# Attention within a chunk of 128 tokens, made as two halves of 64, and y in eight tiles of the TensorE array

## What is computed

```python
# q, k, v, alpha: (batch 4, heads 8, tokens 768, 48)
for t in range(S):
    state = alpha[:, :, t, :, None] * state + einsum('bhd,bhde', k_t, v_t)
    y[:, :, t] = einsum('bhd,bhde->bhe', q[:, :, t], state)
x = y as 3072 tokens x 384
h = x @ w_in;   x = (h * tanh(softplus(h))) @ w_out     # moe, 384 -> 2048 -> 384
h = x @ w_in2;  out = (h * cos(h)) @ w_out2             # moe2, the same shapes
```

## Time and profile before

| | |
|---|---|
| Median of 3 runs | 895.30 us (895.29 to 895.43) |
| The profiled execution, its own time | 896.72 us |
| Its span, first to last instruction | 895.0 us |
| Mean granted TensorE clock | 0.999 of 2.4 GHz |
| PE busy | 882.7 us (99%), 5550 matmuls |
| DVE, ACT, POOL busy | 413.6, 408.7, 371.6 us (46, 46, 42%) |
| Instruction fetch | 0.72 MB in 44 transfers |

### The profile page before, as it was taken

The page is one execution under the profiler, slowest core; times in us unless marked ns, Lnnn a source line. Parts: engine busy times, 40 slices in busy tenths (PEclk is TensorE's granted clock), DMA queues, the critical chain, the costliest instruction groups (busy, mean ns, idle before and its releaser), DMA issues.

```text
span 895.0 us, 13987 instructions
## 1 busy us (share of the span) xinstructions
PE 882.7 (99%) x5550; PEld 729.4 (81%) x5550; DVE 413.6 (46%) x625; ACT 408.7 (46%) x702; POOL 371.6 (42%) x281
## 2 busy tenths in 40 slices
PE   8899999999999999999999999999999999999998
PEld 7688888888888888888878788888888888888886
DVE  8864422222233322221021666565666575666664
ACT  3534332223223222322345765565665565655554
POOL 3686454444444555442355423232323232323333
PEclk9999999999999999999999999999999999999999
DMA  9645221112122211210043200200200200100000
GB/s 212 179 146 146 67 74 40 39 39 75 39 52 59 81 39 40 74 30 1 36 129 101 89 1 0 71 1 1 70 1 1 72 1 0 71 1 1 35 1 36
DMA packets 17153, 48.13 MB, mean 54 GB/s; under 512 B 2752, under 2 KB 2752, under 8 KB 17088
## 3 DMA queue, kind: packets, MB, share of 16 engines
q1 hardware_dynamic: 17088, 47.23, 18.3%
HBM read 37.79 MB, written 9.44 MB: 53 GB/s over the span
## 4 chain that ended last, share of the span: by engine, by line
PE 94%; DVE 2%; DMA 1%; ACT 1%; issue 1%; POOL 0%; ACTq 0%; SPq 0%; DVEq 0%; POOLq 0%
PE bank L444 43%; PE bank L421 43%; PE bank L349 3%; PE bank L370 2%; PE bank L377 1%; PE bank L382 1%; PE bank L393 1%; PE bank L343 1%; DMA shared<-mid 1%; DVE growth L631 1%; DMA shared<-aqk_in 0%; DVE suffix L620 0%; ACT w_hi L486 0%; DVE w_lo L678 0%; ACT g L532 0%
## 5 line engine op out<-in xcount | busy, mean ns | idle before, releaser
L794 POOL TENSOR_TENSOR g_lo<-g,g_hi 128x512 fp32r<-128x512 f32 x192 | 258.3, 1346 | 471.4 <-ACT g_hi L525 471.4
L444 PE MATMUL bank<-g_hi,w_hi 128*128 128x512 f32 x576 | 226.9, 394 | 0.3 <-DVE x_out L694 0.3
L444 PE MATMUL bank<-g_hi,w_lo 128*128 128x512 f32 x576 | 224.3, 389 | 0.0
L525 ACT ACTIVATE g_hi<-g 128x512 fp32r<-128x512 f32 x192 | 120.7, 629 | 131.9 <-PE bank L444 131.2
L421 PE MATMUL bank<-x_hi,w_hi 128*128 128x512 f32 x576 | 162.5, 391 | 3.7 <-ACT g L532 2.2
L444 PE MATMUL bank<-g_lo,w_hi 128*128 128x512 f32 x576 | 166.0, 390 | 0.0
L421 PE MATMUL bank<-x_hi,w_lo 128*128 128x512 f32 x576 | 161.8, 389 | 0.0
L421 PE MATMUL bank<-x_lo,w_hi 128*128 128x512 f32 x576 | 161.8, 389 | 0.0
L421 PEld LDWEIGHTS bank<-x_hi,w_hi 128*128 128x128 f32 x576 | 107.7, 188 | 27.8 <-ACT g L532 3.4
L444 PEld LDWEIGHTS bank<-g_hi,w_hi 128*128 128x128 f32 x576 | 108.1, 188 | 24.8 <-issue 1.1
L539 ACT ACTIVATE shared<-bank 128x512 f32<-128x512 f32 x96 | 57.4, 598 | 154.1 <-PE bank L421 154.1
(11 more groups left out here) (79 smaller groups left out, 625.1 us busy)
## 6 DMA issues: line engine op xcount, KB each, us to landing
w_raw<-w_in SPq DMA_DIRECT2D x32, 384.0 KB, 3.3
shared<-aqk_in SPq DMA_DIRECT2D x44, 192.0 KB, 3.7
v_sb<-v_in SPq DMA_DIRECT2D x24, 256.0 KB, 4.2
shared<-aqk_in SPq DMA_DIRECT2D x48, 96.8 KB, 3.9
mid<-x_out SPq DMA_DIRECT2D x6, 768.0 KB, 5.5
shared<-mid SPq DMA_DIRECT2D x6, 768.0 KB, 6.0
out<-x_out SPq DMA_DIRECT2D x5, 768.0 KB, 4.0
out<-x_out SPq DMA_DIRECT2D x3, 256.0 KB, 2.4
```

What stands on the lines that cost most here:

```text
L444: mm = nc.tensor.matmul(acc[m][:, :], wp[:, f, DM + m * P:DM + (m + 1) * P], gp[:, tile % GB, :], start=(f == 0 and n == 0), stop=(f == FT ...
L525: nc.scalar.activation(g_hi[:, tile % GB, :], g[:, tile % GB, :], ACT.Copy).then_inc(ghi_ready, 1)
L794: nc.gpsimd.tensor_tensor(g_lo[:, tile % GB, :], g[:, tile % GB, :], g_hi[:, tile % GB, :].bitcast(F32), ALU.subtract).then_inc(glo_ready, 1)
```

## The change

A chunk is handled as two halves of 64 tokens. The scores are made within each half alone (64 x 64 instead of 128 x 128; half the masked product is not made any more). What the second half owes to the first comes through the state: `update(c)` now makes the sum of key·value for each half apart and stands ahead of `scores(c + 1)` and y; DVE adds the first half's sum to the state and has the state in the middle (`add_first`, `mid_state`), and later the second half's (`add_second`). y is made by `inner` (v·probs, 32 matmuls) and `outer` (state·q, 16 matmuls, twice), each on 64 rows and 32 columns of the array with 64 moving columns: eight tiles, two row halves by four column groups. The two row halves write different PSUM banks. In the second `outer` they change banks, so it waits for the first (`half_done`), and the transposes of the next chunk's keys (`turn`) stand between. An update is now made for the last four chunks too. The mask is one DVE instruction of the same 512 columns for a chunk, before two. PSUM is laid out anew: `first_product(1)` has a bank of its own, and after a chunk `first_product` waits for the copy of the turned keys instead of the state's addition. The first four chunks get four more ACT copies (`start_state`). `split_x2` comes two steps later, at steps 8, 10 and 12 of a block. Nothing is changed in the 3456 matmuls of the two feed-forward blocks. The diff, cut:

```diff
--- before.py
+++ after.py
...
+def next_scores_at(s):
     c = values_at(s)
     return c + 1 if c is not None and BATCH < c < CHUNKS - 1 else None
...
-    if BLOCKS <= j < 2 * BLOCKS and f in (6, 8, 10):
-        return j, (f - 6) // 2
+    if BLOCKS <= j < 2 * BLOCKS and f in (8, 10, 12):
+        return j, (f - 8) // 2
...
+        mid_state = sb("mid_state", [P, ST])
...
+        def h_of(tile):
+            if tile < TILES:
+                return sc[:, 0, :] if tile == 1 else h0[:, 0, :]
+            return (h0[:, 0, :], sc[:, 0, :], sc[:, 1, :], yu[:, 0, :])[tile % 4]
...
+        def y_of(c):
+            return acc3[:, 0:2, 0:DM // 2] if c in (1, 3) else yu[:, :, 0:DM // 2]
...
+        def update_of(c, half):
+            if half == 1 and c in (2, 3):
+                return acc3[:, 2, (c - 2) * PAIRS * D:(c - 1) * PAIRS * D]
+            return (acc3 if c in (1, 3) else yu)[:, half, DM // 2:DM // 2 + PAIRS * D]
...
+            def turn(c, s):
+                pe.wait_ge(kd_ready, c + 1)
+                if c > 0:
+                    pe.wait_ge(kdt_ready, c)
+                if c == BATCH:
+                    pe.wait_ge(xlo_ready, BATCH)
+                elif c > BATCH:
+                    pe.wait_ge(g_ready, s + 1)
+                for p in range(PAIRS):
+                    mm = nc.tensor.transpose(turn_of(c)[:, p * ROWS:(p + 1) * ROWS], k_of(c)[0:ROWS, p, :],
+                                             ident[0:ROWS, 0:ROWS])
+                mm.then_inc(keys_turned, 1)
...
                 for p in range(PAIRS):
-                    for i in range(2):
-                        rows = slice(64 * i, 64 * i + D)
-                        mm = nc.tensor.matmul((a, b)[i][:, p * P:(p + 1) * P], k_of(c)[rows, p, :],
-                                              q_of(c)[rows, p, :], start=True, stop=True)
-                        if p == PAIRS - 1:
-                            mm.then_inc(scores_done, 1)
...
+                    for half in range(2):
+                        t = slice(HALF * half, HALF * half + HALF)
+                        for i in range(2):
+                            rows = slice(64 * i, 64 * i + D)
+                            mm = nc.tensor.matmul(sc[t, i, p * HALF:(p + 1) * HALF], k_of(c)[rows, p, t],
+                                                  q_of(c)[rows, p, t], start=True, stop=True)
+                mm.then_inc(scores_done, 1)
+            def update(c):
...
+                pe.wait_ge(kdt_ready, c + 1)
...
+                    pe.wait_ge(sum_ready, min(c, UPDATES))
+                for p in range(PAIRS):
+                    for half in range(2):
+                        t = slice(HALF * half, HALF * half + HALF)
+                        for i in range(2):
+                            mm = nc.tensor.matmul(update_of(c, half)[64 * i:64 * i + D, p * D:(p + 1) * D],
+                                                  kd_t[t, c % 2, p, 64 * i:64 * i + D],
+                                                  v_sb[t, c % 3, 2 * p + i, 16 * i:16 * i + D], start=True, stop=True)
+                mm.then_inc(upd_done, 1)
...
+            def inner(c):
+                pe.wait_ge(probs_ready, c + 1)
+                if c >= BATCH:
+                    pe.wait_ge(mid_ready, c - BATCH + 1)
+                else:
+                    pe.wait_ge(first_state, c + 1)
+                for k in range(2):
+                    for half in range(2):
+                        t = slice(HALF * half, HALF * half + HALF)
+                        for n in range(4):
+                            nc.tensor.matmul(y_of(c)[32 * n:32 * n + 32, half, k * HALF:(k + 1) * HALF],
+                                             v_sb[t, c % 3, 2 * n + k, 32 * k:32 * k + 32], probs[t, c % 2, k, n, :],
+                                             start=(k == 0), stop=False, skip_group_check=True)
+                for i in range(2):
+                    for half in range(2):
+                        t = slice(HALF * half, HALF * half + HALF)
+                        for n in range(4):
+                            nc.tensor.matmul(y_of(c)[32 * n:32 * n + 32, half, 2 * HALF:3 * HALF],
+                                             v_sb[t, c % 3, 2 * n + i, 32 - 32 * i:64 - 32 * i], probs[t, c % 2, i, n, :],
+                                             start=False, stop=False, skip_group_check=True)
+            def outer(c, swapped):
+                if c >= BATCH:
...
+                for k in (None, 2):
+                    for i in range(2):
+                        half = 1 - i if swapped else i
+                        if half == 0 and c < BATCH:
+                            continue
+                        ahead = state[:, c % BATCH, :] if half == 0 or c < BATCH else mid_state[:, :]
+                        t = slice(HALF * half, HALF * half + HALF)
+                        rows = slice(64 * i, 64 * i + D)
+                        at = 16 + 16 * i if k is None else 48 - 48 * i
+                        to = (i if k is None else k) * HALF
                         for n in range(4):
...
+                            mm = nc.tensor.matmul(y_of(c)[32 * n:32 * n + 32, half, to:to + HALF],
+                                                  ahead[rows, n * SLAB + at:n * SLAB + at + 32],
+                                                  q_of(c)[rows, n, t], start=False, stop=swapped, skip_group_check=True)
+                mm.then_inc(y_done if swapped else half_done, 1)
+            def values(c, s):
+                inner(c)
+                outer(c, False)
+                ahead = next_scores_at(s)
+                if ahead is not None:
+                    turn(ahead, s)
+                pe.wait_ge(half_done, c + 1)
+                outer(c, True)
...
+                bank = h_of(s)
...
-                c = values_at(s - 1)
-                if c is not None and c < UPDATES:
-                    pe.wait_ge(sum_ready, 2 * (c + 1))
+                c = next_scores_at(s - 1) or (scores_at(s - 1) if s - 1 > 2 else None)
+                if c is not None:
+                    pe.wait_ge(kdt_ready, c + 1)
+                if s == 0:
+                    pe.wait_ge(kdt_ready, BATCH)
+                if s == 1:
+                    pe.wait_ge(probs_ready, BATCH)
...
             def step(s):
+                c = values_at(s)
+                if c == CHUNKS - 1:
+                    update(c)
                 if alive(s):
                     first_product(s)
-                c = scores_at(s)
-                if c is not None:
-                    scores(c)
-                c = values_at(s)
-                if c is not None:
+                if scores_at(s) is not None:
+                    scores(scores_at(s))
+                    turn(scores_at(s), s)
+                if c is not None and c < CHUNKS - 1:
+                    update(c)
+                if c is not None and c > BATCH:
+                    if next_scores_at(s) is not None:
+                        scores(next_scores_at(s))
                     values(c, s)
                 if alive(s - LAG):
                     second_product(s - LAG)
-
...
+                if c == BATCH:
+                    values(c, s)
...
+            def start_state(c):
+                act.wait_ge(state_zero, 2)
+                act.wait_ge(upd_done, c + 1)
+                nc.scalar.activation(dims(state[0:ROWS, c, :]), update_of(c, 0)[0:ROWS, :].rearrange(
+                    "d (p e) -> d p e", p=PAIRS), ACT.Copy).then_inc(first_state, 1)
...
+            def add_first(c):
+                dve.wait_ge(upd_done, c + 1)
+                dve.wait_ge(decayed, c - BATCH + 1)
+                dve.wait_ge(state_zero, 3)
+                if c > BATCH:
+                    dve.wait_ge(y_done, c)
+                nc.vector.tensor_tensor(dims(mid_state[0:ROWS, :]), update_of(c, 0)[0:ROWS, :].rearrange(
+                    "d (p e) -> d p e", p=PAIRS), dims(state[0:ROWS, c % BATCH, :]), ALU.add).then_inc(mid_ready, 1)
+            def add_second(c):
+                dve.wait_ge(y_done, c + 1)
+                dve.wait_ge(xhi_ready, BATCH if c == 1 else c + 1)
+                if c < BATCH:
+                    dve.wait_ge(upd_done, BATCH)
+                ahead = state[0:ROWS, c, :] if c < BATCH else mid_state[0:ROWS, :]
+                nc.vector.tensor_tensor(dims(state[0:ROWS, c % BATCH, :]), update_of(c, 1)[0:ROWS, :].rearrange(
+                    "d (p e) -> d p e", p=PAIRS), dims(ahead), ALU.add).then_inc(sum_ready, 1)
...
                 c = values_at(s)
                 if c is not None:
+                    add_first(c)
+                ahead = next_scores_at(s) or scores_at(s)
+                if ahead is not None:
+                    mask(ahead)
+                p = prepared_at(s)
+                if p is not None:
+                    shrink(p)
+                    grow(p)
+                if c is not None:
+                    keep_x_lo(c)
                     if c < UPDATES:
```

(31 more changed lines are left out.)

238 lines of the change are left out of this document (98 added, 140 removed).

## The result

The changed kernel takes 919.8 us (median of 4 runs, 918.6 to 921.2), the one before 895.3: 1.027 times as long, 95% interval 1.026 to 1.029. The forecast was 879.9, in a range of 874 to 892. The change is slower by 24.5 us. Within the profiled executions it is 23.5 us (spans 918.5 and 895.0).

The account below looks back on a forecast made before the run. PE, busy 99% of the span, bounds the kernel; 11.6 us less in chunks 5 to 18, 2.9 in the start, 0.9 at the end of moe, 15.4 together: 896.72 to 881.3, less 1.4 to the median, 879.9; range 874 to 892.

Parts of the forecast that it names:

- What a chunk is made of: PE's old chunk: transposes, scores, y and update take 3.29 us in rounds of passes, four switches 0.55; 3.84 together.
- The chunk after the change: PE's new chunk: 2.29 us of work and 0.72 of five switches, 3.01 instead of 3.84; 11.6 less in chunks 5 to 18.
- a draw: `inner` on PE waiting for `mid_ready`: 0.66 us against 0.64 of work ahead; worth 0 to 0.3 a chunk, taken as 0.
- the waits show: Rival for chunks: `mid_ready` 0.2 to 0.3 late and dearer tile switches, 0.4 us a chunk, 7.6 in all: 887.5; chance 0.12.
- a period over 20 us: Sign of being wrong: the loop's period of four steps, forecast at 19.4 us instead of 20.2, comes out over 20.
- Together zero: Chunks 19 to 23 and chunk 5's scores and transposes: gains of 0.35 and 0.3 us, losses of 0.2 and 0.4; zero net.
- The start: Before tile 4, with DVE carrying PE: 1.6 us less at tile 3 and 1.3 before tile 4, 2.9 less.
- The end of moe: PE's 0.78 us wait behind ACT's wait for x's DMA goes when x is split two steps later: 0.9 us less.
- The third rival: Chunks' passes themselves bound PE if it can't be fed or start faster than 23 ns: 49 us more, 929; chance 0.10.

Follow-up runs that it names:

- run 1: The changed kernel with `update(c)` ahead of the first product of its step instead of behind it; 912.9 us.
- Run 8: The changed kernel with chunks 0 to 3 made whole as in the kernel before, not in halves, and nothing else; 912.3 us.
- run 2: The changed kernel with DVE's odd w_lo back in its own step, ahead of the scans, as in the kernel before; 915.1 us.
- run 5: The kernel before with only the later split of x (steps 8, 10, 12 instead of 6, 8, 10); 895.4 us, ratio 0.9999.
- run 4: The kernel before with 52 small matmuls (208 instructions), whose results nothing reads, ahead of y in each chunk from 5 on; 924.9 us (one run).
- run 3: The changed kernel with 144 more PE instructions ahead of the first chunk (41 small products, 5 large ones fewer); 921.6 us.
- run 10: The changed kernel with chunks 0 to 3 and 20 to 23 whole, odd w_lo in its step, update ahead of the product only in chunks 4-6 and 12-14; 891.2 us.

## Why the prediction was wrong

Two steps failed above all. The sum had no term for PE's supply of instructions: the rival that named it got 0.10 and a wrong price. And the start was taken as carried by DVE alone. Over the profiled executions the miss is 38.9 us (23.5 and the forecast gain of 15.4): 12.3 in the start, 6.5 behind it at w_lo, 12.2 in chunks 5 to 18, 8.5 in chunks 19 to 23, and 0.6 the other way at the end of moe.

**What a chunk is made of** (right). The rounds, their times and the four switches gave 3.84. By the period it is 3.89: four steps with a chunk take 20.21, without one 16.32 (4 x 4.08).

**The chunk after the change** (right in kind, mis-sized). The forecast was 3.01; measured is 19.70 - 16.32 = 3.38. The update took 0.37 from first to last pass (0.37 forecast) and the scores 0.44 (0.48). Mis-sized were two terms. The 128 passes of y took 0.95 + 0.24 = 1.19 instead of 0.96. The first 32 and the last 32 took 0.24 each, rounds of 0.06 as forecast; the 64 between them (L429 and the first `outer`) took 0.70 instead of 0.48, in rounds of 0.067 to 0.095 and one of 0.163 where L429 begins. What slows these is not shown. And of the gap of 0.31 ahead of `inner`, 0.16 is the wait for `mid_ready` (run 1), which I took as a draw and put at 0: the way back from DVE's add takes 0.14, not 0.05. This is the rival "the waits show", true at nearly its own price: 0.37 a chunk, where it said 0.4. Gained were 0.51 in each undisturbed chunk, some 7 instead of 11.6 us in fourteen. Four stops in these chunks (5.3) and the half clock behind the wait for w_lo (what is left, about 2.4) take it all back and 0.6 more.

My sign of being wrong, a period over 20 us, looked at the loop only, and most periods are 19.70.

**Chunks 19 to 23** (wrong by 8.5). "Together zero" is +2.0 once the stops and the half clock are taken off (periods of 19.74, 19.73, 19.7, 19.98, 18.89 against 19.82, 19.34, 19.32, 19.32, 18.23), because a chunk is 3.38 and not 3.01; three stops add 5.0 and the half clock 1.5.

**The start** (wrong, in sign). Forecast 2.9 less, measured 9.4 more at tile 4. I followed DVE's queue and took PE's four chunks as free of cost between waits; there PE carries the start, with a stop of 3.76 us and 20 us at half clock, and DVE waits for it (1.66 us for scores at 28.3) and is late in turn. The loss is there before the first product: tile 0's starts at 38.14, where it was 27.25 and I had 26.2. Tile 3's is 10.7 late, where I had it 1.6 early; only the 1.3 between tiles 3 and 4 came as forecast. Run 8 gives back 11.8 of it.

**w_lo** (left out). The step of `odd_split_at` I did not cost at all, though it is a moved instruction and stands in the diff: I named what DVE saves, and not what stands ahead of w_lo in its new place, a scan that waits for a DMA. That is 6.5 us of waiting, and in run 2 it is gone.

**The end of moe** (wrong, 0.9 counted twice). The gap was part of the profiled execution's 1.4 over the median. I took it off once as a gain and once as that difference. The changed kernel takes 81.97 us for the stretch that took 82.37 in run 5, so 0.4 is a gain of some other part, which is not shown.

**The third rival** came nearest in size (929 against 919.8) and named "if PE can't be fed", but had the wrong price and place: it spread 23 ns over all passes. y's passes start 9.3 ns apart on average; what costs is the border in three chunks of eight. My grounds against it, starts 7 ns apart in a run of four, show the rate of a burst and say nothing on how long instructions last. The 25 ns of "Back-to-back issue gap" in the Trainium skill's page "TensorE: Matmul & The Clock Gate" do not hold here between different tiles: y's first 32 passes start 7.8 ns apart.

The rule that I had not weighed is on the Trainium skill's page "Advanced Engine Details and Errata", in "ISA Cache": instructions come in lines of 16 KB, 256 instructions, and there are only two lines. The changed kernel's trace agrees on both: 256 per packet, and the first 448 instructions, 192 and a whole 256, have run when the first packet goes out at 16.77. (The same list gives TensorE a larger cache, 128 KB; the stop at number 448 and one packet for each 256 behind it speak against that.) The kernel before shows what was needed to see it: some 188 instructions a chunk, 44 packets, as a rule 0.9 to 1.4 us from issue to landing, against 396 instructions in about 3 us.

## What to carry to other kernels

Count instructions beside array time. A change that halves tiles doubles them. Once the lead from slow instructions was used up, PE's supply here gave 256 instructions in 2.8 us at best (run 4) and mostly in 3.1 to 3.9. A stretch that is denser paid at its second border, unless it was cut by slow instructions such as a product's. Look for idle time put down to "issue" inside a group of equal matmuls, and number the instructions; the same word also stood for a wait on DVE. And an idle time seen in one profiled execution is a gain only if that execution does not stand above the median by as much.

## What the runs showed of the hardware that I had not expected

- PE ran at 1.2 GHz behind some stops and not behind others. In all traces together, none of the stops in the loops under 1.3 us (start to start) was followed by half clock, some of those from 1.3 to 1.8 were (1.58 at 202 in run 1 was, 1.70 at 203 in the changed kernel was not), and all seven of 1.8 and more were. In the loops it lasted 3.4 us each time, in the start up to 17. What decides in between stays open.
- A packet can be late in the start: PE passed its first border at 12.7 us, and the packet went out at 16.8 (before: 15.0 and 18.8). In the chunk at 200 us this took 0.9. It is not always the first packet: in run 3 that one went out before PE passed its first border, and the third took 4.3 us, from 21.3 to 25.6. Whether the DMAs of the start (282 GB/s in that window) are the cause was not tried.
- DVE's w_lo of 0.95 us took 6.30 with POOL at work beside it throughout. In the twelve traces, each w_lo with POOL idle beside it took 0.95 or 0.96, and each that took over 1 us had POOL at work; in runs 1, 3 and 8 the w_lo of piece 7 took 7.1. But POOL's work alone is not enough: some w_lo with POOL busy throughout took 0.93. No run took POOL's part away, so the cause is argued.
- The faster versions scatter more than the kernel before (889.6 to 892.8 in run 10, against 895.3 to 896.3). Run 10's five executions have mean granted clocks of 0.996 to 1.000, the slowest the lowest, so it seems that stops and the half clock behind them come and go; only one execution of each was traced.
